# A convolution and two feed-forward layers on one core: the convolution's steps, x1's last features and layer 2's accumulator waits rearranged

## The reference

```python
out = np.einsum('hk,bskhg->bshg', w, x_unf)      # w: softmax of the taps
h = x @ w_in; g = h * (1.0 / (1.0 + np.exp(-1.702 * h))); x = g @ w_out
h = x @ w_in; P = a[0] + a[1]*h + a[2]*h2 + a[3]*h3
Q = 1.0 + np.abs(b[0]) * np.abs(h) + np.abs(b[1]) * h2
g = P / (Q + 1e-06); out = g @ w_out
```

## Time and profile before

| | |
|---|---|
| median of 3 executions | 1337.24 us (1335.87 to 1340.09) |
| the profiled execution | 1338.71 us, span 1336.9 us, mean granted clock 0.992 |
| PE busy | 1280.2 us (96%) |
| DVE busy | 1131.5 us (85%) |
| ACT busy | 1105.3 us (83%) |
| POOL busy | 535.3 us (40%) |
| DMA | 146.76 MB, mean 110 GB/s |

### The profile page before, as it was taken

One profiled execution on the slowest core, in us unless ns is written; L12 is line 12 of the kernel. 1 busy time (PEld: TensorE's weight loads), 2 busy tenths in 40 slices (PEclk: granted clock), 3 DMA queues, 4 the chain that ended last, 5 costly groups with the idle time before them and its releaser, 6 DMA issues. The chain is left out here.

```text
span 1336.9 us, 15156 instructions
## 1 busy us (share of the span) xinstructions
PE 1280.2 (96%) x5068; PEld 748.1 (56%) x5068; DVE 1131.5 (85%) x1244; ACT 1105.3 (83%) x1280; POOL 535.3 (40%) x387
## 2 busy tenths in 40 slices
PE   5899999999999999999999999999999999999886
PEld 3555565555556555565655556565555656565332
DVE  5648889989888998988898898889889888877886
ACT  5648888888988888898888889888888988888674
POOL 1324443444434344443444444344444434344221
PEclk9999999999999999999999999999999999999898
DMA  7245444544454454454455455544544554454000
GB/s 181 76 97 128 103 122 110 134 110 113 119 120 123 110 134 111 112 124 116 123 111 134 98 121 125 118 122 111 134 107 110 126 119 110 108 125 110 12 1 24
DMA packets 104174, 146.76 MB, mean 110 GB/s; under 512 B 20129, under 2 KB 40609, under 8 KB 104097
## 3 DMA queue, kind: packets, MB, share of 16 engines
q0 software_dynamic: 34560, 62.93, 27.6%
q1 hardware_dynamic: 69060, 82.86, 18.2%
q10 hardware_dynamic: 477, 0.01, 0.0%
HBM read 13.64 MB, written 6.29 MB: 15 GB/s over the span
## 5 line engine op out<-in xcount | busy, mean ns | idle before, releaser
L885 POOL TENSOR_TENSOR work<-work 128x1024 f32<-128x1024 f32 x127 | 305.0, 2401 | 548.9 <-ACT work L565 478.8
L891 POOL DMA_DIRECT2D g_low<-g_nhi x240 | 211.5, 1012 | 190.3 <-DMA g_low<-g 183.8
L746 DVE TENSOR_TENSOR work<-work,h 128x1024 f32<-128x1024 f32 x128 | 156.4, 1222 | 141.0 <-ACT work L565 140.5
L350 PE MATMUL acc_b<-g,down 128*64 128x512 f32 x512 | 248.0, 607 | 22.6 <-DVE g L774 14.3
L330 PE MATMUL acc_a<-g,down 128*128 128x512 f32 x512 | 254.7, 620 | 0.0
L350 PE MATMUL acc_b<-g,down_b 128*64 128x512 f32 x480 | 231.6, 605 | 0.0
L552 ACT ACTIVATE work<-h,par 128x1024 f32<-128x1024 f32 x128 | 142.6, 1114 | 96.7 <-PE h L324 81.6
L316 PE MATMUL h<-x_a_hi,up_a_hi 128*128 128x512 f32 x512 | 208.1, 407 | 13.4 <-DVE x_a_lo L777 5.5
L318 PE MATMUL h<-x_a_hi,up_a_lo 128*128 128x512 f32 x512 | 201.3, 393 | 0.0
L317 PE MATMUL h<-x_a_lo,up_a_hi 128*128 128x512 f32 x512 | 201.1, 393 | 0.0
L319 PE MATMUL h<-x_b,up_b_hi 128*128 128x512 f32 x512 | 200.9, 392 | 0.0
(11 more groups left out here) (124 smaller groups left out, 1952.9 us busy)
## 6 DMA issues: line engine op xcount, KB each, us to landing
g_low<-g SPq DMA_DIRECT2D x240, 256.0 KB, 2.4
g_low<-g_nhi POOLq DMA_DIRECT2D x240, 256.0 KB, 3.7
out<-y_out SPq DMA_DIRECT2D x15, 384.0 KB, 3.0
x_in<-in_x SPq DMA_DIRECT2D x16, 256.0 KB, 3.1
x_in<-in_x SPq DMA_DIRECT2D x32, 64.0 KB, 2.7
work<-in_moe_w_in SPq DMA_DIRECT2D x8, 256.0 KB, 4.4
work<-in_moe_w_in SPq DMA_DIRECT2D x16, 128.0 KB, 4.6
down<-in_moe_w_out SPq DMA_DIRECT2D x4, 384.0 KB, 5.3
```

Of the source, the lines that this page charges most:

```text
L350: return mm(acc_b[l.acc_row:l.acc_row + DB, :], l.down_b[:, f, :], l.g[:, slot, k, :], start=f == 0, stop=f == STEPS - 1)
L746: tt(tu, tu, h, ALU.mult).then_inc(t2_ready, 1)
L885: tt(m, sq[v % 2], seed, ALU.mult).then_inc(m_ready, 1)
L891: pool.dma_start(g_low[:, n % 2, k, :], g_nhi[:, n % 2, k, :], accum_op=ALU.add)\
```

## The change

- x is turned, and copied out, one step later (steps 6 and 7; ACT's copies in steps 5 and 6).
- The 21 convolution instructions stand in four steps: 0 to 7 in step 1, 8 to 11 in step 2, 12 to 15 in step 3, 16 to 20 in step 4. Steps 6 and 7 have none.
- From tile 1 on, ACT rounds `conv_b` in one 128x256 instruction into `x1_hb` (step 5), DVE takes the low part in one into `x1_lb` (step 5), and SP moves four pieces of 64x256 (64 KB each) into `x_b` in step 6, behind that step's L292. `x_a`'s two instructions stand in step 6. PE waits for `x1_b_moved`.
- `acc2_read` becomes `acc2_b_read` and `acc2_a_read`. ACT copies the first half of `acc_b` in step 3 after L571, ahead of L588, the second after L594, and then `acc_a`. PE waits for `acc_b` at the old place and for `acc_a` only ahead of `down_a`.
- DVE makes g's low part for n below 10, and the transfers begin at n = 10.

```diff
-S_XT = (5, 6)
-S_X1_B = 4
-S_X1_A = 5
-S_X1_LO = 5
+S_XT = (6, 7)
+S_X1_B = 5
+S_X1_A = 6
+S_X1_MOVE = 6
...
-    CONV_HEAD = {6: (0, 7), 7: (7, 10)}
-    CONV_AT = (10, 10, 13, 16, NX, NX, NX, NX, NX)
+    CONV_AT = (0, 0, 8, 12, 16, NX, NX, NX, NX)
...
-                if live(n) and n >= DUOS:
+                if live(n) and n >= LAG_UP2:
                     sp.wait_ge(g1_ready, n + 1)
...
+                if s == S_X1_MOVE and tile_live(i + 1):
+                    for done, part, first in ((x1_hb_done, x1_hb, 0), (x1_lb_done, x1_lb, DB)):
+                        sp.wait_ge(done, i + 1)
+                        for half in range(2):
+                            sp.dma_start(L1.x_b[first:first + DB, (i + 1) % 2, half * HALF:(half + 1) * HALF].bitcast(F32),
+                                         part[half * DB:(half + 1) * DB, :].bitcast(F32)).then_inc(x1_b_moved, 16)
...
-                        wait(pe, acc2_read, 3 * (v2 // DUOS))
+                        wait(pe, acc2_b_read, 2 * (v2 // DUOS))
...
                 if live(v2):
+                    if e2 == 0:
+                        wait(pe, acc2_a_read, v2 // DUOS)
                     down_a(e2, slot2).then_inc(g2_used, 1)
...
+                        if i == 0:
+                            pe.wait_ge(x1_b_hi_done, 3)
+                            pe.wait_ge(x1_b_lo_done, 2)
+                        else:
+                            pe.wait_ge(x1_b_moved, 64 * i)
...
+                    wait(act, x1_b_moved, 64 * (tile - 1))
+                    fn(x1_hb[:], conv_b[:], ACT.Copy).then_inc(x1_hb_done, 1)
...
+                if s == S_ACC2 and 0 <= i - 2 < TILES - 1:
+                    act.wait_ge(acc2_b_done, i - 1)
+                    wait(act, y_transposed, 2 * (i - 2))
+                    y_b_half(0)
...
                 if s == S_ACC2 and 0 <= i - 2 < TILES - 1:
+                    y_b_half(1)
                     act.wait_ge(g2_used, DUOS * (i - 1))
-                    wait(act, y_transposed, 2 * (i - 2))
-                    fn(y_b[0:DB, :], acc_b[0:DB, 0:HALF], ACT.Copy).then_inc(acc2_read, 1)
-                    fn(y_b[DB:P, :], acc_b[0:DB, HALF:NT], ACT.Copy).then_inc(acc2_read, 1)
-                    fn(y_a[:], L2.acc_a[:], ACT.Copy).then_inc(acc2_read, 1)
+                    fn(y_a[:], L2.acc_a[:], ACT.Copy).then_inc(acc2_a_read, 1)
...
+                    dve.wait_ge(x1_hb_done, tile)
+                    wait(dve, x1_b_moved, 64 * (tile - 1))
+                    tt(x1_lb[:], conv_b[:], x1_hb[:].bitcast(F32), ALU.subtract).then_inc(x1_lb_done, 1)
...
-                if n < DUOS:
+                if n < LAG_UP2:
                     dve.wait_ge(g1_nhi_ready, n + 1)
...
-                if s == S_X1_LO and tile_live(i + 1):
-                    x1_lo(i + 1, 1 - p)
+                if s == S_X1_B and tile_live(i + 1):
+                    x1_b_lo(i + 1)
+                if s == S_X1_A and tile_live(i + 1):
+                    x1_a_lo(i + 1, 1 - p)
```

More of the change, by code:

```diff
@@ L371, in transpose_y @@
             def transpose_y(tile, half):
-                pe.wait_ge(acc2_read, 3 * (tile + 1))
+                pe.wait_ge(acc2_a_read, tile + 1)
+                pe.wait_ge(acc2_b_read, 2 * (tile + 1))
                 ending = tile == TILES - 1
@@ L418, in downs @@
                         done = down_b(L2, e2, slot2, k)
-                        if last(v2) and k == 1:
+                        if e2 == DUOS - 1 and k == 1:
                             done.then_inc(acc2_b_done, 1)
@@ L524, in x1_a_hi, with x1_b_hi @@
                 fn(L1.x_a_hi[:, p, :], conv_a[:], ACT.Copy).then_inc(x1_a_hi_done, 1)
-            def x1_b_hi(tile, p):
+            def x1_b_hi(tile):
                 act.wait_ge(conv_steps, NX * tile + CONVOLVED)
[L528 to L531, removed]
+                if tile == 0:
+                    fn(L1.x_b[0:DB, 0, 0:HALF], conv_b[0:DB, :], ACT.Copy).then_inc(x1_b_hi_done, 1)
+                    fn(L1.x_b[DB:P, 0, HALF:NT], conv_b[DB:P, :], ACT.Copy).then_inc(x1_b_hi_done, 1)
+                    fn(L1.x_b[0:DB, 0, HALF:NT], conv_b[DB:P, :], ACT.Copy).then_inc(x1_b_hi_done, 1)
+                else:
+                    wait(act, x1_b_moved, 64 * (tile - 1))
+                    fn(x1_hb[:], conv_b[:], ACT.Copy).then_inc(x1_hb_done, 1)
             def weights_hi(l, c, staged, done):
@@ L544, in down_parts, with y_b_half @@
                 fn(down_hi[:, units, :], stage_down[:, units, :], ACT.Copy).then_inc(d1_hi, 1)
+            def y_b_half(half):
+                fn(y_b[half * DB:(half + 1) * DB, :], acc_b[0:DB, half * HALF:(half + 1) * HALF], ACT.Copy)\
+                    .then_inc(acc2_b_read, 1)
             def linear(n, k):
@@ L597, in step @@
                 if ending and n == END:
[L598 removed]
+                    act.wait_ge(acc2_b_done, TILES)
                     act.wait_ge(y_transposed, 2 * (TILES - 1))
[L600 to L601 removed]
+                    y_b_half(0)
+                    y_b_half(1)
                 if s == S_ACC2 and 0 <= i - 2 < TILES - 1:
+                    y_b_half(1)
                     act.wait_ge(g2_used, DUOS * (i - 1))
[L604 to L607 removed]
+                    fn(y_a[:], L2.acc_a[:], ACT.Copy).then_inc(acc2_a_read, 1)
                 if x_turns(n + 1):
@@ L681, in tap @@
                     if k == 0:
-                        wait(dve, (x1_a_hi_done, x1_b_hi_done)[part], (1, 3)[part] * tile)
-                        wait(dve, (x1_a_lo_done, x1_b_lo_done)[part], (1, 2)[part] * tile)
+                        if part == 0:
+                            wait(dve, x1_a_hi_done, tile)
+                            wait(dve, x1_a_lo_done, tile)
+                        elif tile == 1:
+                            dve.wait_ge(x1_b_hi_done, 3)
+                            dve.wait_ge(x1_b_lo_done, 2)
+                        else:
+                            wait(dve, x1_hb_done, tile - 1)
+                            wait(dve, x1_lb_done, tile - 1)
                         return ts(acc[:], src, w, None, ALU.mult)
@@ L706, in conv_ops, with x1_b_lo, x1_a_lo @@
                 return [lambda op=op, done=done: ordered(op, done) for done, op in enumerate(ops)]
[L708 to L714, removed]
+            def x1_b_lo(tile):
+                if tile == 0:
+                    dve.wait_ge(x1_b_hi_done, 1)
+                    tt(L1.x_b[DB:P, 0, 0:HALF], conv_b[0:DB, :], L1.x_b[0:DB, 0, 0:HALF].bitcast(F32), ALU.subtract)\
+                        .then_inc(x1_b_lo_done, 1)
+                    dve.wait_ge(x1_b_hi_done, 2)
+                    tt(L1.x_b[DB:P, 0, HALF:NT], conv_b[DB:P, :], L1.x_b[DB:P, 0, HALF:NT].bitcast(F32), ALU.subtract)\
+                        .then_inc(x1_b_lo_done, 1)
+                else:
+                    dve.wait_ge(x1_hb_done, tile)
+                    wait(dve, x1_b_moved, 64 * (tile - 1))
+                    tt(x1_lb[:], conv_b[:], x1_hb[:].bitcast(F32), ALU.subtract).then_inc(x1_lb_done, 1)
+            def x1_a_lo(tile, p):
                 dve.wait_ge(x1_a_hi_done, tile + 1)
@@ L793, in step @@
                     dve.wait_ge(y_transposed, 2 * (TILES - 1))
-                    nc.vector.tensor_copy(y_a[:], L2.acc_a[:]).then_inc(acc2_read, 1)
+                    nc.vector.tensor_copy(y_a[:], L2.acc_a[:]).then_inc(acc2_a_read, 1)
                 if y_turns(n) == (TILES - 1, 1):
@@ L843, in _ @@
                 .then_inc(w1_lo, 1)
-            x1_lo(0, 0)
+            x1_b_lo(0)
+            x1_a_lo(0, 0)
             dve.wait_ge(setup_act, 3)
```

30 lines of the change are left out of this document (14 added, 16 removed).

## The result

The changed kernel takes **1320.19 us** (median of 4 executions, 1319.97 to 1322.17), the kernel before 1338.1 (4 executions, 1335.87 to 1340.09): a ratio of 0.987, 95% interval 0.9851 to 0.9889. That is 17.9 us less, where 18.95 were forecast (1318.3 us, range 1313.5 to 1326.5). The profiled execution is the slowest of the four, 1322.17 us with a span of 1320.4.

What follows compares the result with a forecast made beforehand. PE, 96% busy, was taken as the bound. Gains of 7.7 + 0.4 + 4.1 + 0.75 + 5.2 + 3.6 less 2.8 lost made 18.95 us: from 1338.71 profiled to 1319.8, or 1318.3 on the median's basis; range 1313.5 to 1326.5.

Steps and rivals of the forecast that it cites:

- Accumulators apart: Step 4 to 5: PE's wait for ACT's L607 goes, 14 x 0.55 = 7.7 us, plus 0.4 us in the tail.
- Convolution out of step 7: Step 1 to 2: PE's wait for DVE's L774 goes, 12 x 0.34 = 4.1 us, plus 0.75 us in tile 2.
- Convolution in four steps: Steps 1 to 3: DVE's longer blocks make PE wait at L350, 0.22 us a tile, 2.8 us lost over 13 tiles.
- rival 1: DVE becomes the bound in steps 1 to 4, each longer block costing 0.2 us more: 1326 us; 15%.
- First tile: PE's steps 5 to 7, held by ACT: 6.1 us gained, less 0.9 for POOL's weight split slowing DVE's taps: 5.2 us.
- ACT's wait for the convolution: Sign of being right: at the start of the run, ACT's wait in front of L517, 7.90 us before, falls below 3 us.
- Rival 2: First tile gives back 4 us less: ACT still holds work ahead of step 6's L569 and the clock falls: 1322 us; 15%.
- Low parts in ten steps: Step 9 to 10: PE's waits at L343 for L891's transfers and the slower matmuls behind them go, 11.46 to 7.84, 3.6 us.
- Transfers of x1: The four SP loads in step 6 stay hidden beside L891's transfers: 0, at most 1 us a tile lost.
- Rival 4: First taps L684, moved to step 1, run beside POOL and cost 2.04 x 13 = 26.5 us: 1345 us, slower; 3%.

Runs made afterwards that it cites:

- experiment 3: The kernel before with only x turned a step later and the convolution in four steps, x1 still copied by the engines: 1330.31 us, 0.994 of before.
- experiment 5: The changed kernel with one more convolution tap in step 2 of every tile (instructions 8 to 12 in place of 8 to 11): 1324.56 us, 0.9903 of before.
- experiment 1: The kernel before with only layer 2's accumulators awaited apart and ACT's copies of them reordered: 1331.5 us, 0.9941 of before.
- experiment 6: The changed kernel with POOL's splits of the second half of w2 one step later in the first tile: 1318.01 us, 0.9856 of before.
- experiment 11: The changed kernel with two more convolution taps in step 2 of every tile (six in place of four): 1363.6 us, 1.0179 of before.

## Why the prediction was right, and where not

The forecast, faster by 18.95 us, held: 17.9. The parts alone, 7.9 + 2.0 + 8.0 us and the 0.9 of the transfers, make 18.8 with an uncertainty of 1 to 2 us each. Step by step:

- **Accumulators apart, 7.7 + 0.4: right.** 0.55 us in step 4 to 5, 7.2 to 7.9 measured. The split between the two halves of the edit wasn't forecast: 0.46 and 0.09.
- **Convolution out of step 7, 12 x 0.34 + 0.75: right.** 9.79 to 9.45 in experiment 3 too, and 0.77 in tile 2 (10.47 to 9.70).
- **Convolution in four steps, 2.8 us lost: wrong, it is nothing.** The step that failed is the adding up of DVE's block. For step 1 I set one more tap, 0.78 us long, behind the end of instruction 6 and came out 0.15 us late. The timeline of the kernel after, end of step 1:

```profile
698.95 0.06 DVE L722 MEMSET halo_a<- 128x6 f32 x1
699.06 0.75 DVE L715 SCALAR_TENSOR_TENSOR conv_a<-xt_a,wts,conv_a 128x512 f32<-128x512 f32 x1
699.06 0.06 DVE L722 MEMSET halo_b<- 64x6 f32 x1
699.76 1.22 DVE L783 TENSOR_TENSOR work<-work,h 128x1024 f32<-128x1024 f32 x1
```

  The tap starts together with the second clear, not behind it, and takes 0.70 to L783: 9.45 from L783 (690.31) to L783. In steps 2 and 3 the blocks last 709.21 to 718.67 = 9.46, where I had 9.48. That DVE then stands exactly at PE's 9.45 was right (experiment 5: one small instruction more and all of it shows), so rival 1 had a real limit in view; but a price worked out to 0.03 us from ends and starts was finer than this method gives.
- **First tile, 5.2: 4.3 in the profiled pair, 2.8 against a trace at full clock** (20.58 of experiment 1 to 17.80). Three terms in it were off. Of the 22.09 us from which the sum started, 1.5 is a fall of the clock that experiment 1 doesn't have. The slowing beside POOL was put at 0.9 us from L787's 1.84 for 1.22; experiment 6 gives it as 1.9 to 2.2. With both, the gain of 6.1 before POOL's price becomes 6.1 - 1.5 - 1.9 = 2.7. And ACT's wait for the convolution stayed at 4.9 us (I had said below 3; experiment 6 has 2.8), since these taps are the ones that POOL holds. Rival 2 named the place. Of the 2.8, moving x brings 1.8 (20.58 to experiment 3's 18.80), and the other 1.0 is the transfers'.
- **Low parts in ten steps, 3.6: too large, the sum of two things.** 7.73 at full clock was forecast as 7.9, but of the 3.7 us gained 1.6 is the clock's, and over many executions 2.0 to 2.7 are left. The prediction had that 1.7 us in rival 2, on the wrong side: as what might remain after, not as what an execution of the kernel before may not lose.
- **Transfers of x1, 0: nearly.** 0 in the middle; L928's transfers land in 3.2 to 6.0 us (median 3.8) as before. In the first tile they save 0.8 to 1.0 us, since ACT does bind there: I had costed ACT's two instructions fewer by the middle of the run alone.
- **Rival 4**, the first taps at 1.5 us, didn't come: L714 takes 0.49 and 0.35 us in all tiles but one. Experiment 11 shows that the danger was real and lay some 0.8 us away (L783, beside which L922 begins, starts 0.76 us after the last tap does), with the last tap of a block in place of the first.

The terms that were too large (first tile and low parts, together 2.5 to 4 us) and the loss that didn't come (2.8) cancel. So it is partly luck that the total is nearer than its parts.

## What to carry to other kernels

Two engines that exclude each other must be read as a pair: when one is moved to the edge of its step, see what the other starts at that edge, for the cost of lateness there is not the lateness but the length of the other's instruction; an extra wait that fixes the order can be the cheaper way. Before a gain is read off one profile, see whether the granted clock in the stretch is the same in another trace with the same code. And cost an engine's relief in the stretch where that engine binds, which in a pipelined kernel can be the first tile alone.

## What the runs showed of the hardware

**DVE and POOL exclude each other by operand, and the order decides.** In the trace of the changed kernel L783 and L785, which read one of their two operands (h) from PSUM, overlap L922 127 and 126 times and always take 1.21 to 1.22 and 1.28 us. L783 came first 108 times and second 19 times, L785 always second. Taps have both operands in SBUF: 2.89 to 2.90 us in all 13 places where L922 came first (experiment 11), 0.74 to 0.75 in the 14 places of the changed kernel where the tap did and L922 started under it. POOL pays in its turn: one L922 that began 0.14 us behind a tap's start took 2.90 us in place of 2.40 (experiment 11). The Trainium skill (SBUF — State Buffer, SBUF: two separate sides) states just this: a shared port pair as an exclusive lock, for a DVE instruction with two SBUF inputs against a GpSimd one that reads SBUF, held for the whole instruction by whoever starts first. The trace agrees: the tap began under POOL's 2.58 us and ended 0.55 us after them. One place of the first tile doesn't fit: L824 began 0.64 us behind POOL's L906 and wasn't held (experiment 6 has the lines). Two operands in SBUF are not the only case: L714 reads one tensor, from SBUF, and took 1.38 us in place of 0.35 where it began 0.13 us behind POOL's L909 (first tile of the changed kernel). My prediction used the sentence on it in the Trainium skill (GPSIMD Engine Reference, 1. Specifications) for the first tile alone. For L885, the later L922, which runs in every step, its rival 4 counted the first taps only, and its rival 1 priced a tap caught by it at 0.2 us, where the runs show nothing when the tap comes first and 2.15 when L922 does.

**The granted clock falls at places that differ between executions of the same code**: 20.58 or 22.09 us for the first tile's steps 5 to 7, 9.87 or 11.46 for step 9 to 10, 33.0 or 34.8 for the end. After the last tile's drain (18.14 us with 12.61 of PE's work) the next stretch took 6.44 us at 0.97 in the kernel before and 8.61 at 0.71 in experiment 1:

```profile
1239.69:1248.30 8.61, 8.61 (x19) 3.52 (x18) 5.74 (x6) 5.89 (x6) 0.72 (x2) 0.71 0.00 1
```

Such falls are 1.5 to 2.2 us each, so one profiled execution can't settle a difference below some 3 us, and the step lengths of the middle can, where the clock is 1.00 in them.
